# Rounding the first expert's weights on GpSimd during attention: parts from unit 10 on, three in every five units, with their loads ahead of V's

## The reference

```python
# 1. attention: 2 batches, 8 heads, 768 tokens, head size 64
scores = q @ k^T / 8; keep = (key < 4) | ((row - key >= 0) & (row - key < 128))
a = exp(masked scores - max); a = a / (sum(a) + 1e-9); x = a @ v
# 2. mixture of experts on 1536 tokens of width 512: 8 experts, w1[e] 512x1024, w2[e] 1024x512
noisy = x @ w_gate + log1p(exp(x @ w_noise)) * noise
top 2 of each token, weights = softmax over the two
out[token] += weight * (relu(x @ w1[e]) @ w2[e])
# 3. dense layer, 512 -> 2048 -> 512
h = x @ w_in; g = h * tanh(softplus(h)); out = g @ w_out
```

## Time and profile before

| what | value |
|---|---|
| median of three runs | 791.1 us (789.21 to 792.53) |
| the profiled execution | 788.75 us, span 787.0 us, mean granted TensorE clock 0.987 |
| PE busy | 759.5 us (97%) |
| PEld busy | 624.9 us (79%) |
| DVE busy | 513.7 us (65%) |
| GpSimd busy | 313.3 us (40%) |
| ACT busy | 285.4 us (36%) |
| DMA | 82.85 MB, mean 105 GB/s |

### The profile page before, as it was taken

The page is one execution under the profiler, slowest core; times in us unless marked ns, Lnnn a source line. Parts: engine busy times, 40 slices in busy tenths (PEclk is TensorE's granted clock), DMA queues, the critical chain, the costliest instruction groups (busy, mean ns, idle before and its releaser), DMA issues.

```text
span 787.0 us, 13211 instructions
## 1 busy us (share of the span) xinstructions
PE 759.5 (97%) x4198; PEld 624.9 (79%) x4199; DVE 513.7 (65%) x897; ACT 285.4 (36%) x594; POOL 313.3 (40%) x330
## 2 busy tenths in 40 slices
PE   8999939999999999999999999989999999999997
PEld 5888737888888888888888888767888888888886
DVE  6789964454454544545445454468998888878776
ACT  6988713030302103021030300355554555554443
POOL 5599827555651816518174827621011020000000
PEclk9999978999999999999999999999999999999999
DMA  6575664626450724507244534010000110010001
GB/s 204 161 246 181 170 219 141 194 100 197 139 167 32 237 67 138 166 30 238 67 135 158 172 108 134 27 54 27 27 27 27 54 45 11 0 54 1 0 1 53
DMA packets 49485, 82.85 MB, mean 105 GB/s; under 512 B 18080, under 2 KB 22240, under 8 KB 49440
## 3 DMA queue, kind: packets, MB, share of 16 engines
q1 hardware_dynamic: 31440, 33.89, 13.1%
q10 hardware_dynamic: 13600, 33.96, 13.1%
q0 software_dynamic: 4400, 14.42, 6.4%
HBM read 66.01 MB, written 16.25 MB: 105 GB/s over the span
## 4 chain that ended last, share of the span: by engine, by line
PE 88%; DVE 7%; ACT 2%; issue 2%; DMA 0%; POOL 0%; DVEq 0%; ACTq 0%; POOLq 0%
PE bank L1308 22%; PE bank L1297 22%; PE bank L1369 16%; PE bank L1350 15%; PE bank L1281 3%; PE bank L1202 3%; PE bank L1177 2%; PE bank L1274 2%; PE bank L1186 2%; PE bank L1211 1%; ACT probs L660 1%; DVE bank L838 1%; PE bank L1161 1%; PE bank L1342 1%; DVE kT L861 0%
## 5 line engine op out<-in xcount | busy, mean ns | idle before, releaser
L565 POOL TENSOR_TENSOR wgt<-stage,wgt 128x1024 f32 (+1 forms) x64 | 151.2, 2401 | 107.5 <-ACT wgt L724 107.4
L1308 PE MATMUL bank<-wgt,hT 128*128 (+1 forms) x744 | 186.1, 399 | 0.0
L1297 PE MATMUL bank<-wgt,xT 128*128 (+1 forms) x744 | 182.3, 394 | 1.5 <-DVE xT L1043 1.5
L1297 PEld LDWEIGHTS bank<-wgt,xT 128*128 128x128 f32 x744 | 137.3, 188 | 29.0 <-DVE xT L1043 1.8
L724 ACT ACTIVATE wgt<-stage 128x1024 f32 (+1 forms) x64 | 61.6, 1045 | 270.0 <-PE bank L1308 259.8
L1308 PEld LDWEIGHTS bank<-wgt,hT 128*128 128x128 f32 x744 | 135.1, 188 | 25.9
L1369 PE MATMUL bank<-wgt,gT 128*128 128x512 f32 x576 | 141.1, 394 | 4.8 <-DVE gT L1104 4.8
L1350 PE MATMUL bank<-x2T,wgt 128*128 128x512 f32 (+1 forms) x588 | 138.2, 385 | 0.9 <-DVE x2T L1081 0.9
L1369 PEld LDWEIGHTS bank<-wgt,gT 128*128 128x128 f32 x576 | 108.3, 190 | 28.6 <-DVE gT L1104 6.1
L1350 PEld LDWEIGHTS bank<-x2T,wgt 128*128 128x128 f32 x588 | 108.7, 188 | 23.0 <-POOL wgt L637 1.1
L1049 DVE TENSOR_SCALAR h<-bank 128x512 f32<-128x512 f32 x62 | 42.9, 691 | 65.1 <-PE bank L1297 65.1
(11 more groups left out here) (165 smaller groups left out, 922.1 us busy)
## 6 DMA issues: line engine op xcount, KB each, us to landing
stage<-in_moe_w ACTq DMA_DIRECT2D x48, 512.0 KB, 3.6
stage<-in_moe_w SPq DMA_DIRECT2D x16, 512.0 KB, 5.8
y_dram<-y_sb SPq DMA_DIRECT2D x31, 256.0 KB, 2.4
stage<-in_moe_w_in ACTq DMA_DIRECT2D x8, 512.0 KB, 4.5
stage<-in_moe_w_out ACTq DMA_DIRECT2D x8, 512.0 KB, 4.1
v_in<-in_v SPq DMA_DIRECT2D x8, 384.0 KB
x_dram<-x_sb SPq DMA_DIRECT2D x16, 192.0 KB, 3.0
out<-o_sb SPq DMA_DIRECT2D x12, 256.0 KB, 2.1
```

The costliest lines, as they stand in the source:

```text
L565: nc.gpsimd.tensor_tensor(cols(parity, 1, u * UNIT, UNIT), stage[:, u, :], cols(parity, 0, u * UNIT, UNIT).bitcast(fp32), ALU.subtract).th ...
L1297: ins = T.matmul(HA[half][:], xT[:, a, c, :], cols(par, b, c * F + half * 512, 512), start=c == 0 and n == 0, stop=c == NC - 1 and n == 2)
L1308: ins = T.matmul(YB[kk % 2][:], hT[:, a, c, :], cols(par, b, NC * UNIT + c * DM, DM), start=c == 0 and n == 0, stop=c == F // P - 1 and n ...
```

## The change

Three edits. `WEIGHTS_FROM` goes from 14 to 10, the period of a weight unit from 4 to 5 attention units, and the parts lie at offsets 0, 1 and 3 of the period rather than at 0, 1 and 2. Weight unit w then has its parts at 10+5w, 11+5w and 13+5w; the last is at 48, which the loop of GpSimd (n up to 48) reaches in its last step. On SyncE the two weight loads of an iteration are sent behind Q's and K's and ahead of the wait for V's, no longer behind V's and the stores.

```diff
-        WEIGHTS_FROM = 14
+        WEIGHTS_FROM, WEIGHT_UNITS, WEIGHT_PARTS = 10, 5, (0, 1, 3)
...
                 if i + 1 < NP:
                     sp.wait_ge(qk_ready, 4 * i)
                     load_qk(i + 1, (i + 1) % 2)
+                for u in range(2 * (i - 2), min(2 * (i - 1), UNITS)):
+                    src, to = unit_of(0, u)
+                    sp.dma_start(to, src).then_inc(unit_loaded[u], 16)
                 sp.wait_ge(pv_ready, QT * (i - 1))
                 load_v(i, i % 2)
                 store_x(i - 2)
-
-                for u in range(2 * (i - 2), min(2 * (i - 1), UNITS)):
-                    src, to = unit_of(0, u)
-                    sp.dma_start(to, src).then_inc(unit_loaded[u], 16)
...
                 for u in (n, n + 1):
-                    if u >= WEIGHTS_FROM and (u - WEIGHTS_FROM) // 4 < UNITS and (u - WEIGHTS_FROM) % 4 < 3:
-                        first_set((u - WEIGHTS_FROM) // 4, (u - WEIGHTS_FROM) % 4)
+                    unit, part = (u - WEIGHTS_FROM) // WEIGHT_UNITS, (u - WEIGHTS_FROM) % WEIGHT_UNITS
+                    if 0 <= unit < UNITS and part in WEIGHT_PARTS:
+                        first_set(unit, WEIGHT_PARTS.index(part))
```

## The result

The changed kernel took 785.11 us in the median of five runs (784.67 to 788.08), the kernel before 791.1 us (788.79 to 792.53). The ratio is 0.9948, with a 95% interval of 0.9924 to 0.9973: faster by half a per cent. The forecast was 786.7 us and a gain of 4.4; the medians differ by 6.0. The profiled execution took 786.44 us, with a span of 784.7 us.

What follows compares the result with a forecast made beforehand. It took DVE, its remainders held by GpSimd's subtracts, to bound attention's second half. Values of 44 5.1 us earlier, less 0.7 for routing pieces, gave 4.4 us: 791.1 to 786.7 us, range 784.6 to 791.2.

Steps and rivals of the forecast that it cites:

- The bound: Attention's second half: DVE slips through remainders stretched by GpSimd's subtracts, 9.2 us of added DVE time; 4.1 us not TensorE's own.
- Steps 1 and 2: Steady attention: lighter GpSimd load, 1.47 us a step from 1.84; of ten steps with collisions two stay, costing nothing.
- Rival B: Attention: the collisions stay, DVE remains the bound, only about 1.0 us gained, 790.1 us; chance 0.14.
- Steps 3 and 4: Late attention: values of 44 come 5.1 us earlier, less 0.7 for DVE's routing pieces, leaving 4.4 us.
- the term of 0.7 us for DVE's routing pieces: Attention from u = 36 to 46: DVE just keeps pace, so 0.7 us is taken off the gain, range 0.3 to 1.2.
- Step 5: Last attention steps: the subtracts in 46 and 48 stay covered, cost 0, ceiling 2.3 us.
- Rival E: Last attention steps: GpSimd still behind, cuts late, up to 2.3 us slower, 793.4 us, at most 794.7; chance 0.07.
- Step 6: Weight loads sent earlier arrive in time without delaying V; cost 0, from 0 to 1 us; stores also cost 0.
- rival F: Attention: a weight load is late, GpSimd waits ahead of its cuts, the change does nothing, 791.1 us; chance 0.06.
- Step 7: Behind attention: routing, gather and slots move rigidly by 4.4 us; profiled execution 784.35, median 786.7 us.
- Rival C: Slot 0: clock rises late, about 3.4 us at half speed costs 1.7 us, leaving 788.4 us; chance 0.10.
- rival D: Whole kernel: the 0.7 isn't lost and the clock rises early, 5.1 us and up to 1 more, 785.2 us; chance 0.08.

Runs made afterwards that it cites:

- e3_write_only: Kernel before with GpSimd's 16 subtracts replaced by write-only fills about as long, the first expert's remainders left out: 785.67 us, ratio 0.9956.
- e5_early_dense: Changed kernel with period 4 instead of 5 and parts at offsets 0, 1, 2, so the old density begun four units earlier: 789.1 us, ratio 0.9992.
- e0_changed: The changed kernel measured again, with no edit: 786.92 us, ratio 0.9947 to the kernel before.
- e6_spread: Changed kernel with its 24 parts laid by a list, steps 8 to 40, then 46 and 48, none in 42 and 44: 786.6 us, ratio 0.9934.
- e1_loads_only: Kernel before with only the weight loads moved ahead of V's, GpSimd's parts as they were: 789.1 us beside 788.96, ratio 1.0009.
- e2_parts_only: Changed kernel with the weight loads put back behind V's and the stores, so only the parts are moved: 791.71 us, ratio 1.0033 to the kernel before.
- e7_fill_gap: Changed kernel with five filling matmuls on TensorE between the first tokens' transposes and slot 0: 785.26 us, ratio 0.9925 to the kernel before.
- e10_changed_fill: Changed kernel with five filling matmuls ahead of slot 0, tested beside the kernel before with the same fills: 784.69 us, ratio 0.9943.

## Why the prediction was right

**The bound.** The reading that DVE and not GpSimd held TensorE, through remainders stretched by collisions, is shown: taking the subtracts' reads away while GpSimd stays full (e3_write_only) gives the same pace as the change, and no piece of the chain between 49 and 94 us was GpSimd's.

**Steps 1 and 2, density and phase.** The remainders' mean was forecast near 0.65 and is 0.64. Lowering the density is what brings the phase: the early start alone leaves it at 1.01 (e5_early_dense). Rival B was the fate of e5_early_dense, not of the change. That only two steps would collide was too neat. Steps 22 and 32 hold half of what remains (1.2 of 2.4 us, by the durations of the 18 remainders against those in e3_write_only); the other half is spread over five more steps, 0.2 to 0.3 us each. TensorE's pace didn't notice up to u = 42. GpSimd's idle time rose from 0.2 to 0.44 us a step (7.16 us over the same stretch), where 0.57 was forecast.

**Steps 3 and 4, the sum.** The scores of 46 were forecast at 89.9 and came at 90.33. The values of 44 were put 5.1 us earlier and came 3.7 earlier. So the term of 0.7 us for DVE's routing pieces was mis-sized; it measured 1.4 to 1.5, above its own range of 0.3 to 1.2. The place was right, its cause partly missed: I had counted the held L921 as freed, and the cast of step 44 held its neighbour L913 for 1.02 us instead (L921 for 1.01 in e0_changed). Without parts in these steps the indices come 0.4 to 0.7 us earlier (e6_spread).

**Step 5, the last steps.** Right: the two subtracts there cost nothing; the values of 46 follow those of 44 by 2.80 us, as before. Rival E didn't come.

**Step 6, the loads.** Cost 0 was right (e1_loads_only), and the earlier loads are a condition of the rest: without them the parts at unit 10 make the kernel slower than before (e2_parts_only, ratio 1.0033). I had put this as rival F; the move of the loads is what shut it out.

**Step 7 and the clock.** The block behind attention did not move rigidly in every run. Rival C named slot 0 at the low clock and a price of 1.7 us; the profile shows 1.6. But its mechanism was wrong: the clock isn't late to rise, it falls again behind TensorE's wait for the first tokens. The change doesn't cause this. The profile of the kernel before has no such fall (4.39 us for slot 0's matmuls), but e3_write_only, on the old schedule, has one (5.99 us), and so has e5_early_dense with the old density (5.97 us), while e0_changed, the changed kernel itself, has none (4.42 us). What decides whether a given execution has it stays open. The 3.4 us at half speed, from which C had its price, stood in none of the prediction's rows; the price came near all the same.

**The number.** That the measured 785.11 us lies in the range owes something to luck. The sum of step 4 was 0.7 us too high for the values of 44 (4.4 against 3.7). The forecast proper was a gain of 3.3 to 5.1 us, 786.0 to 787.8; the medians differ by 6.0, about what rival D has (785.2), though D's first condition didn't hold (the 0.7 was lost twice over) and its early clock brought 0.35 us. The rest is the scatter of the clock: of the kernel before, three of five runs lay in its upper heap, of the changed one a single run. Step 7 put the median 2.35 us above the profiled execution; for the changed kernel it lies 1.3 below it. The medians differ by 4.3 beside e0_changed (791.18 to 786.92), and by 4.0 where the gap is filled. The forecast of 4.4 was for this last quantity, and that agreement is hardly luck: the values of 44, the token indices and slot 0 come 3.7, 3.75 and 4.1 us earlier. The lower end of the range, 784.6, is not reached by D's own terms either, which end at 785.0 (791.1 - 5.1 - 1).

The upper heap lies 3.3 to 3.5 us above the lower, twice the 1.6 of slot 0 in the profile. The profile of e6_spread, 2.9 us above that of e0_changed, has the fall in slot 0 (1.4 us) and a longer one behind the wait in the dense layer (1.3 us). The changed kernel's own two profiles, 786.44 and 784.8 us, differ by the fall in slot 0 alone, 1.6 us. That both falls together make the upper heap is likely, but no profile of a run of this kernel in that heap exists to show it.

The version that beats both in these runs is the changed kernel with five fills: 785.26 and 784.69 us in its two tests. Against the changed kernel without them the lesser scatter is the surer part of its gain.

## What to carry to other kernels

An engine that looks full may be innocent: look at whether the instructions of its neighbour grow when it works (here 0.53 to 1.02 us), and at what those have in common. GpSimd's casts and subtracts, which read SBUF, cost DVE instructions with two SBUF inputs what was left of their length here; spread so that most of them ended before DVE got there, the same work cost almost nothing up to u = 42. When a consumer in a fixed queue is moved earlier, look at its loads first (e2_parts_only). And compare the granted clock of the runs before a gain of half a per cent is read from two medians: here five short fills ahead of slot 0 took out the runs of the changed kernel above 786 us.

## What the runs showed of the hardware that I had not expected

- A DVE instruction on 128x48 elements, 0.21 us alone, takes 1.02 us when a GpSimd cast starts 0.07 us ahead of it, and one on 128x6 elements, 0.17 us alone, 1.27 us beside a subtract. What it costs is the length of the GpSimd instruction, not its own.
- Fills on GpSimd (128x512, 0.53 us each) didn't hold DVE: the remainders are back at 0.53 us with GpSimd 92% busy (54.92 of 59.9).
- The hold works both ways: beside a remainder of 0.77 us a cut on GpSimd took 0.73 us in the kernel before, 0.41 alone; the mean of its kind went from 0.52 to 0.43 where the subtracts were fills.
- In the profile of the changed kernel the granted clock, at 0.88 and 0.97 in the windows from 120 to 124 us, in which TensorE worked 1.1 and 1.04 us of 2, was 0.50 in the next one, and the longest wait in them was 1.51 us. With five filling matmuls of 1.40 us in that wait it stayed at 1.0, in e7_fill_gap's and e10_changed_fill's profiles. Behind the stand of 3.69 us in e2_parts_only, and behind TensorE's wait of about 4 us in the dense layer (3.89 to 4.05 us), which all twelve profiles have, it was 0.5 as well.
